# Turning the attention output one tile at a time through the last two heads, and casting its plain blocks on GpSimd

## The chip, the cores and the metric

One core of a Trainium2 chip runs the kernel. The metric is the device time of one execution in microseconds (us). TensorE (PE) multiplies matrices, VectorE (DVE) and ScalarE (ACT) work on SBUF and PSUM, GpSimd (POOL) on SBUF only, and SyncE (SP) issues most of the DMAs. Each engine works through its own instructions in order and waits on semaphores for the others.

## The reference, cut to what matters

```
# attention: 2 batches x 8 heads, 768 tokens, 64 wide; keys of the query's own hash bucket only
scores = np.where(q_bucket == k_bucket, scale * q @ k.T, -1e9)
attn = exp(scores - max) / (sum + 1e-9);  attn_out = attn @ v
x = attn_out.transpose(0, 2, 1, 3).reshape(1536, 512)
# dense mixture: every expert on every token, P from 8 Sinkhorn rounds over x @ w_gate
out = sum_e P[:, e:e+1] * (np.maximum(x @ w1[e], 0) @ w2[e])
# then a routed mixture: one expert a token, on out
```

## The kernel before

**Attention.** The 16 heads are worked in 8 pairs (`pair(j, first, last)`), each of 12 steps `s`, a step being one tile of 128 queries; `i` counts the 96 steps. In step `i` TensorE computes the scores of step `i+2`, transposes the probabilities of step `i` and multiplies those of step `i-1` by V. ScalarE takes the exponential of step `i` (`exp`, L801) and then copies the transposed probabilities of step `i-1` as fp16 (L808). VectorE subtracts for their low halves (`take_probsT_lo`, L1107) and takes the row maximum of step `i+2` (L1113), which the exponential of that step needs. The scores of step `i+2` wait for the exponential of step `i`, since they share a bank of PSUM.

**Turning x.** The dense mixture multiplies with x transposed, in two batches `b` of six tiles of 128 tokens each. `turn_x(t)` has four PE transposes of one tile (L1661) into a PSUM bank, and `take_xf(t)` copies them to `xf` (L843 on ScalarE, L1164 on VectorE). Batch 0 holds heads 0 to 7, which are complete long before the last pair. All of its tiles go through one bank, so each turn waits for the copy of the tile before. In the last pair the steps 6, 7 and 8 turn two tiles each: one between the scores and the transposes, one at the end of the step.

**Seven blocks.** The dense first layer uses Strassen-like sums: seven products per group (`group_product`), of seven sums of W1 blocks and of x blocks. Blocks 0, 4 and 6 of x are plain quarters of `xf`; blocks 2, 1, 3 and 5 are sums that GpSimd makes (`sum_x`, L697 to L705, in that order). Each block needs a high half in fp16 (`x7_hi`, an ACT copy, L854) and a low half (`x7_lo`, a subtraction, L710 on GpSimd for the plain blocks and L1190 on VectorE for the sums). In expert 0 the products of group 0 wait for the blocks of batch 0 one by one, those of group 4 for batch 1.

**Groups.** An expert has 8 groups `g` of 7 products, each product of 6 matmuls (L1722, L1724, L1725). For each group VectorE adds parts out of PSUM: L1275 first (product 5 of the group waits for it), then L1372 for the group before, L1279, L1283, L1286, L1287 and L1290. Batch 1 (tiles 6 to 11) is turned in the groups 0 and 1 of expert 0 through two banks, so tile `t` waits for the copy of tile `t-2`. Its ScalarE work stands in `second_x(g, place)`, between the copies of those groups.

**Splitting W1.** During the attention GpSimd also splits V (`split_v`) and the first expert's W1 (`split_first_w1`), multiplying by a scale that lies in SBUF and is broadcast along the row (`v_scale`, `w_scale`), as a `tensor_tensor`.

## Time and profile before

| | |
|---|---|
| median of 3 runs | 1354.65 us (1350.77 to 1355.5) |
| the profiled execution's own time | 1356.91 us |
| its span, first to last instruction | 1355.1 us |
| PE busy | 97% of the span |
| DVE, ACT, POOL busy | 63%, 42%, 23% |
| granted TensorE clock, mean | 0.993 of full speed |

Busy shares are of the span. With PE at 97%, the time is PE's work and the few stretches in which it waits. The change touches the stretch from about 219 us (last pair of heads) to about 287 us (group 3 of expert 0).

### The profile page before, as it was taken

The page shows a single profiled execution, that of the slowest core. Times are in us where ns is not written, and L with a number is a line of the kernel's source. Part 1 is how long each engine was busy: PE and PEld are TensorE (multiplying, and loading weights), DVE is VectorE, ACT ScalarE, POOL GpSimd, SP SyncE. Part 2 cuts the span into 40 slices and gives each one's busy share as a digit, 9 for nine tenths or more (in the row PEclk, how much of TensorE's full clock was granted, in tenths as well). Part 3 has the DMA queues.
Part 4 walks back from the last instruction along what each step waited for, and adds up shares of the span by engine and source line. Part 5 has one row for each costly group of instructions (what it writes and reads, how often), then busy time and mean ns, then how long its engine had stood idle before and what let it go on. Part 6 is the DMA issues. An engine that isn't in the chain of part 4 may idle for free.

```text
span 1355.1 us, 24730 instructions
## 1 busy us (share of the span) xinstructions
PE 1318.6 (97%) x9435; PEld 763.7 (56%) x9435; DVE 848.4 (63%) x1491; ACT 569.7 (42%) x870; POOL 305.5 (23%) x229
## 2 busy tenths in 40 slices
PE   6999999899999999999999999999999999998987
PEld 3776767665455456445545644654564465556665
DVE  5999999786576247436634742753464275567983
ACT  5999999652134114304312420440242043226662
POOL 4787776522002100300300030030003000121211
PEclk9999999999999999999999999999999999998989
DMA  9345441051011011001101100200110112468940
GB/s 235 95 100 124 111 110 36 37 204 62 1 62 63 1 62 62 0 0 66 58 0 62 62 0 28 72 23 0 62 62 0 62 63 78 180 205 281 342 151 21
DMA packets 51631, 109.84 MB, mean 81 GB/s; under 512 B 5216, under 2 KB 8840, under 8 KB 51568
## 3 DMA queue, kind: packets, MB, share of 16 engines
q1 hardware_dynamic: 48880, 105.40, 24.6%
q0 software_dynamic: 2240, 3.35, 0.7%
q8 instruction: 45, 0.74, 0.2%
q10 hardware_dynamic: 448, 0.19, 0.1%
q14 instruction: 18, 0.15, 0.0%
HBM read 93.57 MB, written 17.34 MB: 82 GB/s over the span
## 4 chain that ended last, share of the span: by engine, by line
PE 89%; DVE 4%; ACT 3%; issue 2%; DMA 1%; SPq 1%; POOL 0%; ACTq 0%; POOLq 0%; DVEq 0%
PE ps L1696 14%; PE ps L1699 14%; PE ps L1700 14%; PE ps L1722 11%; PE ps L1724 11%; PE ps L1725 11%; PE ps L1617 5%; PE ps L1605 2%; PE ps L1607 2%; PE ps L1589 2%; PE ps L1627 1%; PE ps L1629 1%; PE ps L1631 1%; ACT probsT_hi L808 1%; ACT probs L801 1%
## 5 line engine op out<-in xcount | busy, mean ns | idle before, releaser
L1722 PE MATMUL ps<-x_hi,w_hi 128*128 128x384 f16 x896 | 292.3, 326 | 2.3 <-DVE parts L1275 1.2
L1724 PE MATMUL ps<-x_lo,w_hi 128*128 128x384 f16 x896 | 292.3, 326 | 0.0
L1725 PE MATMUL ps<-x_hi,w_lo 128*128 128x384 f16 x896 | 292.3, 326 | 0.0
L1699 PE MATMUL ps<-w_lo,h 128*128 128x512 f16 x768 | 291.2, 379 | 0.0
L1700 PE MATMUL ps<-w_hi,h 128*128 128x512 f16 x768 | 291.2, 379 | 0.0
L1696 PE MATMUL ps<-w_hi,h 128*128 128x512 f16 x768 | 291.1, 379 | 0.0
L1332 DVE SCALAR_TENSOR_TENSOR x<-ps,gate_now,x 128x512 f32<-128x512 f32 x84 | 63.1, 751 | 251.6 <-PE ps L1700 250.6
L938 ACT ACTIVATE x1s<-ps 128x384 f32<-128x384 f32 x64 | 30.4, 475 | 326.5 <-PE ps L1725 326.5
L636 POOL TENSOR_TENSOR wf<-wf 128x1024 f32<-128x1024 f32 x8 | 18.8, 2355 | 633.1 <-PE ps L1725 622.4
L955 ACT ACTIVATE h<-parts 128x1152 f16<-128x1152 f32 x64 | 74.4, 1163 | 140.2 <-DVE parts L1290 140.2
L1700 PEld LDWEIGHTS ps<-w_hi,h 128*128 128x128 f16 x768 | 75.1, 98 | 90.6
L1696 PEld LDWEIGHTS ps<-w_hi,h 128*128 128x128 f16 x768 | 75.7, 99 | 86.3
L1699 PEld LDWEIGHTS ps<-w_lo,h 128*128 128x128 f16 x768 | 75.1, 98 | 86.3
L1722 PEld LDWEIGHTS ps<-x_hi,w_hi 128*128 128x128 f16 x896 | 87.7, 98 | 61.1 <-DVE x_lo L1190 1.7
L1725 PEld LDWEIGHTS ps<-x_hi,w_lo 128*128 128x128 f16 x896 | 87.7, 98 | 57.9
L1724 PEld LDWEIGHTS ps<-x_lo,w_hi 128*128 128x128 f16 x896 | 87.7, 98 | 57.8
L1107 DVE TENSOR_TENSOR probsT_lo<-ps,probsT_hi 128x384 f16<-128x384 f32 x192 | 97.9, 551 | 11.6 <-ACT probsT_hi L808 10.2
L801 ACT ACTIVATE probs<-ps,row_bias,row_scale 128x768 f32<-128x768 f32 x96 | 95.2, 992 | 1.6 <-DVE row_bias L1122 0.8
L1113 DVE TENSOR_REDUCE row_max<-ps 128x1 f32<-128x768 f32 x96 | 91.1, 949 | 3.8 <-PE ps L1607 3.8
L1372 DVE SCALAR_TENSOR_TENSOR h<-parts,h 128x1152 f16<-128x1152 f32 x64 | 86.8, 1356 | 10.4 <-ACT h L955 10.4
L1617 PE MATMUL ps<-const,probs 128*128 128x128 f32 x576 | 87.1, 285 | 3.5 <-DVE probsT_lo L1107 2.3
L808 ACT ACTIVATE probsT_hi<-ps 128x384 f16<-128x384 f32 x192 | 83.4, 490 | 8.6 <-PE ps L1617 7.5
(229 smaller groups left out, 2270.3 us busy)
## 6 DMA issues: line engine op xcount, KB each, us to landing
wf<-w1a SPq DMA_DIRECT2D x32, 512.0 KB, 6.0
w_stage_in<-w2a SPq DMA_DIRECT2D x8, 2048.0 KB, 8.7
w_in<-w1b SPq DMA_DIRECT2D x4, 2048.0 KB, 9.5
w_in<-w2b SPq DMA_DIRECT2D x4, 2048.0 KB, 9.8
w_in_b<-w1b SPq DMA_DIRECT2D x4, 2048.0 KB, 10.0
w_in_b<-w2b SPq DMA_DIRECT2D x4, 2048.0 KB, 10.2
rows<-blank SPq DMA_DIRECT2D x1, 6682.0 KB, 21.5
qk_in<-kT SPq DMA_DIRECT2D x32, 192.0 KB, 4.3
```

Source lines behind the costliest of these rows:

```text
L801: act.activation(probs[r][:, :], psS[r], ACT.Exp, bias=row_bias[:, slot:slot + 1], scale=row_scale[:, slot:slot + 1]).then_inc(probs_ready, 1)
L808: act.activation(probsT_hi[r][:, half * HALF:(half + 1) * HALF], psT[half], ACT.Copy).then_inc(probsT_hi_ready, 1)
L1107: dve.tensor_tensor(probsT_lo[r][:, keys], psT[half], probsT_hi[r][:, keys], ALU.subtract).then_inc(probsT_lo_ready, 1)
L1113: dve.tensor_reduce(row_max[:, slot:slot + 1], psS[r], AX.X, ALU.max).then_inc(max_ready, 1)
L1372: dve.scalar_tensor_tensor(out=h[:, b, 1, i, 1:4, :], in0=now[:, :, :], scalar=0.0, in1=h[:, b, 0, i, 1:4, :], op0=ALU.max, op1=ALU.subtra ...
L1617: last = pe.transpose(psT[half][:, k * P:(k + 1) * P], probs[r][:, keys], ident)
L1696: first = pe.matmul(acc, a_hi, b_hi, start=(m == 0), stop=False)
L1699: pe.matmul(acc, a_hi, b_lo, start=False, stop=False)
L1700: last = pe.matmul(acc, a_lo, b_hi, start=False, stop=(m == n - 1))
L1722: pe.matmul(group_bank(g, role), w_hi, x_hi, start=(opens and kt == 0), stop=False, skip_group_check=not opens)
L1724: pe.matmul(group_bank(g, role), w_hi, x_lo, start=False, stop=False, skip_group_check=not opens)
L1725: last = pe.matmul(group_bank(g, role), w_lo, x_hi, start=False, stop=(kt == 1), skip_group_check=not opens)
```

## The change

It has five parts.

1. Batch 0's tiles are turned one a step, in the steps 0, 2, 3, 4, 5 and 6 of the last pair, each between that step's scores and its transposes. ScalarE takes all of them; VectorE takes none.
2. ScalarE casts only the four sums, at the steps 8 to 11. GpSimd casts the plain blocks 0, 4 and 6 itself and then subtracts.
3. VectorE makes the low halves of the blocks 2 and 1 in the steps 10 and 11, of 3 and 5 after the last step. GpSimd's `normalise` of head 14 moves between the sums.
4. Tiles 10 and 11 of batch 1 are turned after the second product of group 1 (before: after the fifth), and ScalarE takes them one place sooner. In batch 1 GpSimd casts and subtracts block 0, makes the four sums, then casts and subtracts the blocks 4 and 6.
5. The scalings of V and W1 on GpSimd use constants in the instruction (`tensor_scalar`) and no broadcast operand.

```diff
-X_HI = (0, 4, 6, 2, 1, 3, 5)
-X_LO_DVE, X_LO_POOL = (1, 2, 3, 5), (0, 4, 6)
-TAKEN_BY_DVE = (1, 3, 4, 5)
+X_SUMS, X_BLOCKS = (2, 1, 3, 5), (0, 4, 6)
+TURNED_AT = (0, 2, 3, 4, 5, 6)
...
-                pool.tensor_tensor(w7_hi[:, k, :, :], wf[:, k, :, :], scale, ALU.mult).then_inc(w1_hi_ready, 1)
+                pool.tensor_scalar(w7_hi[:, k, :, :], wf[:, k, :, :], W_SCALE, 1.0, ALU.mult, ALU.mult
+                                   ).then_inc(w1_hi_ready, 1)
...
-            def x7_lo_part(b, k):
-                pool.wait_ge(x7_hi_ready, x_hi_count(b, k))
+            def split_x_block(b, k):
+
+                n = len(X_BLOCKS) * b + X_BLOCKS.index(k) + 1
+                pool.wait_ge(xf_ready, QT * b + (QT if k == 6 else QT // 2))
+                pool.tensor_scalar(x7_hi[:, b, k, :, :], x_block(k, b), 1.0, 1.0, ALU.mult, ALU.mult
+                                   ).then_inc(x7_hi_pool, 1)
+                pool.wait_ge(x7_hi_pool, n)
                 pool.tensor_tensor(x7_lo[:, b, k, :, :], x_block(k, b), x7_hi[:, b, k, :, :], ALU.subtract
                                    ).then_inc(x7_lo_pool, 1)
...
             def sum_and_split_x(b):
 
-                x7_lo_part(b, 0)
-                x7_lo_part(b, 4)
+                split_x_block(b, 0)
+                if b == 0:
+                    split_x_block(b, 4)
                 sum_x(b)
-                x7_lo_part(b, 6)
+                if b > 0:
+                    split_x_block(b, 4)
+                split_x_block(b, 6)
...
-                    if last and s >= QT:
-                        first_x(s - QT)
+                    if last and s in TURNED_AT:
+                        take_xf(TURNED_AT.index(s))
+                    if last and s >= 2 * QT - 4:
+                        x7_hi_part(0, s - 2 * QT + 4)
...
-                    if turns_x:
-                        turn_x(2 * (s - QT))
+                    if last and s in TURNED_AT:
+                        turn_x(TURNED_AT.index(s))
...
-                    if turns_x:
-                        turn_x(2 * (s - QT) + 1)
...
+                    if first and g == 1:
+                        turn_x(QT + 4)
+                        turn_x(QT + 5)
                     bank_free(2)
```

On ScalarE, the rows of the last pair of heads around step 6, before: L801 is an exponential, L808 the two copies of transposed probabilities, L843 a turned tile's copy, L854 a cast.

```order
L801 ACTIVATE probs<-ps,row_bias,row_scale 128x768
L808 ACTIVATE probsT_hi<-ps 128x384 x2
L801 ACTIVATE probs<-ps,row_bias,row_scale 128x768
L808 ACTIVATE probsT_hi<-ps 128x384 x2
L843 ACTIVATE xf<-ps 128x4x128
L801 ACTIVATE probs<-ps,row_bias,row_scale 128x768
L808 ACTIVATE probsT_hi<-ps 128x384 x2
L823 ACTIVATE denom<-ps,eps_bias 128x6
L825 ACTIVATE o_sum<-ps 128x384
L843 ACTIVATE xf<-ps 128x4x128
L854 ACTIVATE x_hi<-xf 128x768
```

And the same stretch of the changed kernel (L796 is its exponential, L803 the copies of probabilities, L838 the copy of a turned tile, L844 a cast of a sum):

```order
L796 ACTIVATE probs<-ps,row_bias,row_scale 128x768
L803 ACTIVATE probsT_hi<-ps 128x384 x2
L838 ACTIVATE xf<-ps 128x4x128
L796 ACTIVATE probs<-ps,row_bias,row_scale 128x768
L803 ACTIVATE probsT_hi<-ps 128x384 x2
L838 ACTIVATE xf<-ps 128x4x128
L796 ACTIVATE probs<-ps,row_bias,row_scale 128x768
L803 ACTIVATE probsT_hi<-ps 128x384 x2
L818 ACTIVATE denom<-ps,eps_bias 128x6
L820 ACTIVATE o_sum<-ps 128x384
L796 ACTIVATE probs<-ps,row_bias,row_scale 128x768
```

The copies of tiles now stand one to a step, from the first step of the pair on, each ahead of the next step's exponential; the casts of the plain blocks are gone from this engine.

On VectorE, the end of the last pair and the start of group 0, before: L1190 are the low halves of the sums.

```order
L1107 TENSOR_TENSOR probsT_lo<-ps,probsT_hi 128x384 x2
L1113 TENSOR_REDUCE row_max<-ps 128x1
L1118 TENSOR_SCALAR row_scale<-row_max 128x1
L1122 TENSOR_SCALAR row_bias<-row_max,row_scale 128x1
L1107 TENSOR_TENSOR probsT_lo<-ps,probsT_hi 128x384 x6
L1190 TENSOR_TENSOR x_lo<-x_sums,x_hi 128x768 x4
L1135 TENSOR_SCALAR denom<-ps 128x6
L1129 RECIPROCAL denom<-denom 128x6
L1138 TENSOR_TENSOR x_attn<-ps,denom 128x6x64
L1275 TENSOR_TENSOR parts<-ps,x1s 128x384
```

In the changed kernel (L1086 are the low halves of the probabilities, L1143 those of the sums):

```order
L1086 TENSOR_TENSOR probsT_lo<-ps,probsT_hi 128x384 x2
L1092 TENSOR_REDUCE row_max<-ps 128x1
L1097 TENSOR_SCALAR row_scale<-row_max 128x1
L1101 TENSOR_SCALAR row_bias<-row_max,row_scale 128x1
L1086 TENSOR_TENSOR probsT_lo<-ps,probsT_hi 128x384 x2
L1143 TENSOR_TENSOR x_lo<-x_sums,x_hi 128x768
L1086 TENSOR_TENSOR probsT_lo<-ps,probsT_hi 128x384 x2
L1143 TENSOR_TENSOR x_lo<-x_sums,x_hi 128x768
L1086 TENSOR_TENSOR probsT_lo<-ps,probsT_hi 128x384 x2
L1143 TENSOR_TENSOR x_lo<-x_sums,x_hi 128x768 x2
L1114 TENSOR_SCALAR denom<-ps 128x6
L1108 RECIPROCAL denom<-denom 128x6
```

Two of the four now stand ahead of probabilities that TensorE multiplies.

On GpSimd, batch 1, before: L710 subtracts for a plain block, L697 to L705 are the sums, and the first row holds three subtractions, of block 6 of batch 0 and of the blocks 0 and 4 of batch 1.

```order
L710 TENSOR_TENSOR x_lo<-xf,x_hi 128x768 x3
L697 TENSOR_TENSOR x_sums<-xf 128x768
L700 TENSOR_TENSOR x_sums<-xf,x_sums 128x768
L703 TENSOR_TENSOR x_sums<-xf,x_sums 128x768
L705 TENSOR_TENSOR x_sums<-xf 128x768
L710 TENSOR_TENSOR x_lo<-xf,x_hi 128x768
L724 ISA
```

In the changed kernel (L699 casts, L702 subtracts, L682 to L692 are the sums; the first two rows are block 0 of batch 1, and the views write `x_hi` and `x_lo` for `x7_hi` and `x7_lo`):

```order
L699 TENSOR_SCALAR x_hi<-xf 128x768
L702 TENSOR_TENSOR x_lo<-xf,x_hi 128x768
L682 TENSOR_TENSOR x_sums<-xf 128x768
L685 TENSOR_TENSOR x_sums<-xf,x_sums 128x768
L690 TENSOR_TENSOR x_sums<-xf,x_sums 128x768
L692 TENSOR_TENSOR x_sums<-xf 128x768
L699 TENSOR_SCALAR x_hi<-xf 128x768
L702 TENSOR_TENSOR x_lo<-xf,x_hi 128x768
L699 TENSOR_SCALAR x_hi<-xf 128x768
L702 TENSOR_TENSOR x_lo<-xf,x_hi 128x768
L719 ISA
```

A cast has come in ahead of each subtraction, and behind the sums there are two blocks, four instructions, where there was one instruction.

## Rows read from the trace of the kernel before

**Rows 1.** The page: each engine's busy time, share of the span, instructions.
```profile
PE 1318.6 (97%) x9435; PEld 763.7 (56%) x9435; DVE 848.4 (63%) x1491; ACT 569.7 (42%) x870; POOL 305.5 (23%) x229
```

**Rows 2.** Stretches: length; busy PE, PEld, DVE, ACT, POOL (instructions); clock; DMA share, GB/s.
```profile
233.00:247.50 14.50, 12.31 (x160) 9.79 (x157) 13.16 (x31) 11.75 (x23) 6.60 (x5) 1.00 0.43 146
247.50:257.00 9.50, 7.03 (x87) 5.03 (x88) 7.63 (x9) 6.26 (x12) 7.14 (x4) 1.00 0.01 2
```

**Rows 3.** PE in order of time: start, duration; scores, first turned tile, first product.
```profile
220.49 0.39 PE L1605 MATMUL ps<-K,Q 76*128 76x512 f16 x1
222.86 0.38 PE L1605 MATMUL ps<-K,Q 76*128 76x512 f16 x1
225.09 0.38 PE L1605 MATMUL ps<-K,Q 76*128 76x512 f16 x1
234.01 0.38 PE L1605 MATMUL ps<-K,Q 76*128 76x512 f16 x1
234.67 0.60 PE L1661 MATMUL ps<-const,x_attn 128*128 128x128 f32 x4
236.84 0.39 PE L1605 MATMUL ps<-K,Q 76*128 76x512 f16 x1
243.67 0.38 PE L1605 MATMUL ps<-K,Q 76*128 76x512 f16 x1
252.33 0.33 PE L1722 MATMUL ps<-x_hi,w_hi 128*128 128x384 f16 x1
255.59 0.34 PE L1722 MATMUL ps<-x_hi,w_hi 128*128 128x384 f16 x1 [1.15 <-DVE x_lo L1190]
```

**Rows 4.** ACT in order of time, step 6 of the last pair, and a later cast.
```profile
235.31 0.60 ACT L843 ACTIVATE xf<-ps 128x512 f32<-128x512 f32 x1 [1.12 <-PE ps L1661]
235.80 0.99 ACT L801 ACTIVATE probs<-ps,row_bias,row_scale 128x768 f32<-128x768 f32 x1
246.71 0.84 ACT L854 ACTIVATE x_hi<-xf 128x768 f16<-128x768 f32 x1
```

**Rows 5.** POOL and DVE in order of time, at the end of the attention.
```profile
250.55 1.86 POOL L705 TENSOR_TENSOR x_sums<-xf 128x768 f32<-128x768 f32 x1
252.37 2.35 POOL L710 TENSOR_TENSOR x_lo<-xf,x_hi 128x768 f16<-128x768 f32 x1
251.80 3.73 DVE L1190 TENSOR_TENSOR x_lo<-x_sums,x_hi 128x768 f16<-128x768 f32 x2
```

**Rows 6.** In order of time, group 1 of expert 0: third product, copies of tiles 8, 9.
```profile
264.18 0.33 PE L1722 MATMUL ps<-x_hi,w_hi 128*128 128x384 f16 x1
264.22 1.07 ACT L843 ACTIVATE xf<-ps 128x512 f32<-128x512 f32 x2
```

**Rows 7.** POOL and DVE in order of time, groups 2 and 3 of expert 0.
```profile
269.86 2.17 POOL L697 TENSOR_TENSOR x_sums<-xf 128x768 f32<-128x768 f32 x1
276.83 2.19 POOL L705 TENSOR_TENSOR x_sums<-xf 128x768 f32<-128x768 f32 x1
278.97 1.65 POOL L710 TENSOR_TENSOR x_lo<-xf,x_hi 128x768 f16<-128x768 f32 x1
278.14 0.96 DVE L1294 CAST earlier<-const 128x128 bf16<-128x128 f32 x1
279.02 1.63 DVE L1296 CAST x<-const 128x12 uint32<-128x12 f32 x1
280.63 1.81 DVE L1190 TENSOR_TENSOR x_lo<-x_sums,x_hi 128x768 f16<-128x768 f32 x2
```

**Rows 8.** POOL by line: count, busy us and mean ns, idle before.
```profile
L581 POOL TENSOR_SCALAR marks<-hashed,mark_top,mark_floor 44x768 f16<-44x768 f32 x15 | 14.7, 981 | 11.1 <-ACT hashed L816 10.1 <-issue 1.0
L663 POOL TENSOR_TENSOR w_hi<-wf,w_scale 128x1024 f16<-128x1024 f32 x7 | 13.2, 1893 | 0.3
L604 POOL TENSOR_TENSOR V_hi<-V_in,v_scale 128x384 f16<-128x384 f32 x16 | 13.9, 869 | 34.0 <-PE ps L1631 23.0 <-DMA V_in<-v 10.2 <-POOL marks L581 0.7
```

**Rows 9.** Who PE waited for, 225 to 290 us: total, times, longest.
```profile
PE ps L1722 <- DVE parts L1275: 1.2, 1, 1.2
```

More of the change, by code:

```diff
@@ L348, in x_tile @@
             return xf[:, t // QT, :, (t % QT) * P:(t % QT + 1) * P]
-        def act_tiles(t):
-            return sum(u not in TAKEN_BY_DVE for u in range(t + 1))
-        def dve_tiles(t):
-            return sum(u in TAKEN_BY_DVE for u in range(t + 1))
-        def x_hi_count(b, k):
-            return NP * b + X_HI.index(k) + 1
         def group_bank(g, role):
@@ L683, in _ @@
                 split_first_w1(j - 1)
-            normalise(G - 2)
             pool.wait_ge(v_split, 3 * G)
@@ L1170, in pair @@
                     g, r, q = 2 * j + s // QT, s // QT, s % QT
-                    if last and s in (QT + 1, QT + 2, QT + 3):
-                        take_xf((1, 3, 5)[s - QT - 1])
                     if not (first and s == 0):
@@ L1175, in pair @@
                         take_probsT_lo(i - 1, 1, (s - 1) % 2)
-                    if last and s == QT + 2:
-                        take_xf(4)
+                    if last and s >= 2 * QT - 2:
+                        x7_lo_part(0, X_SUMS[s - 2 * QT + 2])
                     ends_head = q == 1 and not (first and s == 1)
@@ L1667, in pair @@
                     g, r, q = 2 * j + s // QT, s // QT, s % QT
-                    turns_x = last and QT <= s < QT + 3
                     if not (last and s >= 2 * QT - 2):
@@ L1761, in expert @@
                     group_product(g, 0, 1, 4, False)
-                    if first and g < 2:
-                        turn_x(QT + 4 * g)
-                        turn_x(QT + 4 * g + 1)
+                    if first and g == 0:
+                        turn_x(QT)
+                        turn_x(QT + 1)
                     pe.wait_ge(u2_ready, groups_done + 1)
```

80 lines of the change are left out of this document (31 added, 49 removed).

## The prediction

> **What bounds the kernel now.** The page comes first: PE is busy for 97% of the span [rows 1], so only two things can move the time, PE's own work and PE's waits. The change takes nothing from PE: it still turns 12 tiles, and multiplies the same blocks. So I look for waits, in the stretch that the change touches, with the busy time by stretches. PE lacks 2.19 us in 233 to 247.5 and 2.47 us in 247.5 to 257 [rows 2]; from 225 to 290 the list of waits has one of 1.2 us more, for L1275 [rows 9]. Together 5.9 us, 0.43% of the time, is all that the change could win there. The order of PE in time then shows where each loss lies [rows 3].
>
> From 225.09 to 234.01, four steps without a turned tile, a step takes 2.23 us. Step 6, the first with tiles, takes 2.83 (234.01 to 236.84), and the next two take 6.83 together (to 243.67). The first product of expert 0 starts at 252.33. Two products later PE stands, for 1.15 us by the row, until 255.59: it waits for the low half of a sum.
>
> **The turned tiles of batch 0.** What does one tile a step cost? Step 6 of before has its first tile just where the change puts each of its tiles, and the rows follow one another without a gap: scores 0.66 us (234.01 to 234.67), the tile's transposes 0.60, ScalarE's copy at 235.31, the exponential at 235.80 for 0.99, and the next step's scores at 236.84 [rows 3, 4]. ScalarE works in order: it has the copy ahead of the next exponential, and so the exponential can't start before PE has done scores and tile. The chain is 2.83 us against 2.23, so 0.60 a tile, although ScalarE and PE both have time left in a step. Step 0 took 2.37 (220.49 to 222.86), it grows by 0.46. Steps 2 to 5 grow by 4 x 0.60 = 2.4. Step 6 stays. PE is at step 7 about 2.9 us late.
>
> Steps 7 and 8 hold no tile now. Before they took 6.83. Step 1, which like step 7 copies a head's sums, took 2.23 (222.86 to 225.09) [rows 3]; I take 2.3 for step 7, and for step 8, whose ScalarE row has a cast of 0.84 [rows 4] beside the exponential and two copies, 2.4. That gives 2.1 back. From step 9 to the first product it took 8.66 us (243.67 to 252.33). ScalarE now has a cast in each of the steps 9, 10 and 11 where it had two, and VectorE has two low halves of about 0.9 us (1.81 for two [rows 7]) ahead of probabilities that PE waits for. I put 0.3 on it; nothing to 1.5 is open. First product: 2.9 - 2.1 + 0.3 = 1.1 us later.
>
> The wait of 1.15 us after it goes: blocks 2 and 1 have their low halves before the last probabilities are done, block 3 follows 0.9 us later, and PE needs it only after three products. First term: 1.1 - 1.15 = **0.0 us**, with -2.9 and +1.2 as its ends (the tiles free, or the tail 1.5).
>
> **Tiles 10 and 11.** Tile 10 now stands behind two products of group 1, which end at 264.18, and each tile waits for the copy of two tiles before. ScalarE copies tiles 8 and 9 from 264.22 for 1.07 us [rows 6], so the first is there at about 264.8 and the second at 265.3. Unhindered, tile 11 would start by 264.18 + 0.60 = 264.8 at the latest. Nothing of this waits before. Second term: **+0.6 us** (0.5 to 0.8), and ScalarE can't be quicker, since its copies stand behind work of group 0 that keeps its distance to PE.
>
> **GpSimd and VectorE in batch 1.** GpSimd and VectorE hold one another up. At 251.80 VectorE starts two low halves, which take 3.73 us for the 1.81 of the pair at 280.63 [rows 5, 7]. The first can only end after GpSimd's sum (250.55 + 1.86 = 252.41), the second after its subtraction (to 254.72), which itself takes 2.35 for 1.65. In groups 2 and 3 the casts at 278.14 and 279.02 end with GpSimd's instructions too (279.02 and 280.62), and behind them stand the low halves and L1275, for which PE waited 1.2 us [rows 7, 9].
>
> The Trainium skill says the same (GPSIMD Engine Reference, section 8, Key points): GpSimd contends with VectorE instructions that have two SBUF inputs or run in a two-port mode. It speaks against this change, which gives GpSimd three more instructions in each batch; the rows agree with it.
>
> Before, GpSimd is done at 280.62, just as VectorE comes to its two low halves. How long is it busy now? The cast is not in the trace. A tensor_scalar of 768 elements took 0.98 us on 44 partitions [rows 8], a tensor_tensor of the same size up to 1.65; I take 1.0, being the same kind of instruction. By the Trainium skill (the same page, 3.1) one-input work runs at 1.03 cycles an element at 1.2 GHz: an estimate of 0.7 us, which would take 0.9 us from GpSimd's queue. Block 0 can start with tile 8's copy at about 265.3, cast and subtraction end near 268.2, the four sums took 9.1 (269.86 to 278.97) [rows 7] and end near 277.3, and two blocks of 1.0 + 1.65 bring it to 282.6 or, with what VectorE takes, 284. So both low halves of 0.9 fall under a busy GpSimd: each waits for the rest of an instruction, 0 to 1.65, on average about 0.7, so +1.4. The casts of before waited for longer instructions (2.19 and 1.65); now some are of 1.0, -0.4. PE already stands there, so all of it counts. Third term: **+1.0 us** (-0.5 to +2.8).
>
> **What costs nothing.** The scalings with a constant go from 1.89 us and 0.87 [rows 8] to perhaps 1.3 and 0.6. GpSimd is ahead in the attention: it waits for PE 23.0 us in all before L604. If that cover is gone they cost (below). Batch 0's blocks: turned by step 3, the blocks 0 and 4 are cast and subtracted by about 237, the sums start with the sixth copy near 239 and are made by 247, each ahead of ScalarE's cast. Even a cast of 1.65 would leave that so.
>
> **Sum.** 0.0 + 0.6 + 1.0 = +1.6 us. Against the profiled execution's 1356.91 (its span 1355.1) that is 1358.5; it lies 2.3 above the median of the three runs, so on the median 1354.65 + 1.6 = 1356.2 us.
>
> **Rivals.**
> - *The tiles are free.* A step has slack on ScalarE and PE, and if the copy slips into it the 2.9 us do not arise: -1.3 in all, 1353.3 us. For it: one tile is less than the slack of two engines together. Against it: the 2.83 of step 6, which has the same order. 0.20.
> - *Contention rules.* All low halves in batch 1, and those of the steps 10 and 11 too, wait a whole GpSimd instruction: third term 2.8, tail 1.5, +4.6 in all, 1359.2 us. For it: the 3.73. By the rule of the Trainium skill above (GPSIMD Engine Reference, Key points) this is the case to expect. 0.17.
> - *All waits go*, the 5.9 us: 1348.8 us. Against it: the chain and tile 10. 0.04.
> - *GpSimd becomes the bound (slower).* The two-constant multiplication may be dearer than the multiplication with a broadcast operand. A pair of heads has two such instructions on W1 and four on V, 2 x 1.89 + 4 x 0.87 = 7.3 us, and GpSimd waits for PE 23.0 / 8 = 2.9 a pair. From 1.4 times the duration it decides; at 1.6 times it is 4.4 - 2.9 = 1.5 us a pair, 10 us in the seven, 1366 us. Against it: 0.98 for 768. 0.07.
> - *As forecast*, 0 to +3: 0.52.
>
> **How the numbers follow.** The bounds of the terms give -1 to +5 in the likeliest case; the free tiles reach down to 1353, and three runs of the same kernel lie 4.7 us apart. I take 1350.5 to 1361.0, which leaves out the fourth rival, the third, and the ends of the spread. A measurement of this kernel tells about 0.5% (6.8 us) from no change. Faster by that is below 1347.9, which even the third rival doesn't reach: 0.03. Slower by that takes the GpSimd rival or the contention at its worst with the spread: 0.09. Within: 0.88.
>
> **What would show it.** Scores 2.83 us apart in the steps 0 and 2 to 6 (2.23: the tiles are free). First product near 1 us later against the last pair's start, and no wait for a low half behind it. A wait of PE before tile 11 of 0.5 to 0.8. GpSimd busy to about 284 in batch 1, and the wait for L1275 in group 3 of 2 us, not 1.2. A cast on GpSimd of about 1.0 us. I am wrong if casts or constant scalings take over 1.65, or if PE waits at group 4 for a block that GpSimd makes last.

## The result, and the profile after

| | before | changed |
|---|---|---|
| median, 18 runs each | 1354.61 us (1350.77 to 1357.26) | 1358.11 us (1354.67 to 1360.76) |
| ratio, 95% interval | | 1.0025 (1.0016 to 1.0034) |
| profiled execution, its span | 1356.91, 1355.1 us | 1360.46, 1358.6 us |

The change costs 3.5 us, 0.25% of the time. That is within the 0.5% that the prediction called no change, but the interval of the ratio excludes 1, so it is a small loss. The prediction said +1.6.

The page of the changed kernel, each engine's busy time, share and instructions. PE has the 97% of [rows 1] still; GpSimd (POOL) is busy for 16 us less.

```profile
PE 1319.1 (97%) x9435; PEld 764.0 (56%) x9435; DVE 848.0 (62%) x1487; ACT 566.6 (42%) x868; POOL 289.3 (21%) x235
```

PE of the changed kernel in order of time (start, duration). L1577 is the scores (L1605 before), L1634 a turned tile (L1661), L1692 the first product of a block (L1722), L1666 the second layer. These rows answer to [rows 3, 6].

```profile
220.65 0.39 PE L1577 MATMUL ps<-K,Q 76*128 76x512 f16 x1
221.32 0.60 PE L1634 MATMUL ps<-const,x_attn 128*128 128x128 f32 x4
223.49 0.39 PE L1577 MATMUL ps<-K,Q 76*128 76x512 f16 x1 [0.31 <-ACT probs L796]
225.86 0.38 PE L1577 MATMUL ps<-K,Q 76*128 76x512 f16 x1
226.53 0.60 PE L1634 MATMUL ps<-const,x_attn 128*128 128x128 f32 x4
228.70 0.39 PE L1577 MATMUL ps<-K,Q 76*128 76x512 f16 x1 [0.37 <-ACT probs L796]
...
240.13 0.39 PE L1577 MATMUL ps<-K,Q 76*128 76x512 f16 x1 [0.31 <-ACT probs L796]
244.74 0.38 PE L1577 MATMUL ps<-K,Q 76*128 76x512 f16 x1
251.42 1.51 PE L1589 MATMUL ps<-const,probs 128*128 128x128 f32 x6 [1.81 <-DVE probsT_lo L1086]
255.09 0.51 PE L1692 MATMUL ps<-x_hi,w_hi 128*128 128x384 f16 x1
267.47 0.82 PE L1634 MATMUL ps<-const,x_attn 128*128 128x128 f32 x5 [0.52 <-ACT xf L838]
320.07 0.38 PE L1666 MATMUL ps<-w_hi,h 128*128 128x512 f16 x1
```

Three stretches follow from such rows, and the experiments below are read by the same three: the last pair of heads from its first scores to those of step 9 (**steps**), from there to the first product of expert 0 (**tail**), and from it to the first product of the second layer (**first layer**; it starts at 315.23 before). Their sum is the time that the change can touch. The changed kernel was traced a second time, later, with the median of its own in the last table.

| us | steps | tail | first layer | sum |
|---|---|---|---|---|
| before | 23.18 | 8.66 | 62.90 | 94.74 |
| changed | 24.09 | 10.35 | 64.98 | 99.42 |
| changed, second trace | 24.08 | 8.55 | 65.35 | 97.98 |

The sum grows by 4.7 us in one trace and by 3.2 in the other; the medians differ by 3.5.

Who PE waited for in the changed kernel, 220 to 325 us (total, times, longest). Before there was one wait of 1.2 us in the first layer that the list gives [rows 9], beside the low half's 1.15 [rows 3]. The low half is gone. In its place stand a wait of 1.8 us in the tail, two of 0.6 for x1s, one of 1.1 for the bank that L1247 frees (L1275 before) and one of 0.5 for the copies of the tiles 8 and 9.

```profile
PE ps L1589 <- DVE probsT_lo L1086: 3.4, 5, 1.8
PE ps L1577 <- ACT probs L796: 2.0, 6, 0.4
PE ps L1692 <- ACT x1s L917: 1.2, 2, 0.6
PE ps L1692 <- DVE parts L1247: 1.1, 1, 1.1
PE ps L1634 <- ACT xf L838: 0.5, 1, 0.5
```

Stretches of the changed kernel: length, busy time of PE, PEld, DVE, ACT and POOL, the granted clock, then DMA. The first two answer to [rows 2], where the clock was 1.00 in both. Here it is 0.67 in the second, and the short stretches show where: it is full at 250.50 and half, 1.2 in place of 2.4 GHz, from 250.75 on, inside the wait of 1.81 us (249.61 to 251.42), and it is full again by 257.50. The transposes that start there take 1.51 us; the same six took 0.92 at full clock.

```profile
233.00:247.50 14.50, 12.74 (x171) 9.77 (x169) 12.44 (x30) 13.30 (x25) 11.24 (x9) 1.00 0.39 138
247.50:257.00 9.50, 6.87 (x73) 5.47 (x74) 8.78 (x13) 4.37 (x8) 2.40 (x2) 0.67 0.01 2
...
250.25:250.50 0.25, 0.00 (x0) 0.00 (x0) 0.25 (x1) 0.25 (x1) 0.00 (x0) 1.00 0.00 0
250.75:251.00 0.25, 0.00 (x0) 0.00 (x0) 0.25 (x2) 0.13 (x1) 0.00 (x0) 0.50 0.00 0
...
250.00:252.00 2.00, 0.58 (x3) 0.61 (x4) 2.00 (x4) 0.88 (x2) 0.00 (x0) 0.66 0.00 0
252.00:254.00 2.00, 1.92 (x23) 1.70 (x21) 1.67 (x4) 0.98 (x2) 0.00 (x0) 0.50 0.00 0
254.00:256.00 2.00, 1.89 (x21) 1.42 (x22) 1.97 (x5) 0.00 (x0) 0.00 (x0) 0.50 0.03 8
256.00:258.00 2.00, 2.00 (x9) 1.05 (x8) 0.64 (x2) 0.49 (x1) 0.00 (x0) 0.63 0.00 0
```

POOL by line in the changed kernel (count, busy us and mean ns): V's scaling took 869 ns before and W1's 1893 [rows 8], now 540 and 1046; the cast is L699. GpSimd's new instructions are shorter than the ones they replace, and the new cast takes 1.07 in the mean.

```profile
L590 POOL TENSOR_SCALAR V_hi<-V_in 128x384 f16<-128x384 f32 x16 | 8.6, 540 | 38.8 <-PE ps L1603 27.9 <-DMA V_in<-v 10.5 <-POOL A L581 0.2
L648 POOL TENSOR_SCALAR w_hi<-wf 128x1024 f16<-128x1024 f32 x7 | 7.3, 1046 | 0.4
L699 POOL TENSOR_SCALAR x_hi<-xf 128x768 f16<-128x768 f32 x6 | 6.4, 1068 | 17.5 <-ACT xf L838 17.5
```

### The profile page after: what moved, and what is told of

Same layout as the page of the kernel before. It is cut to its first block, busy times and chain, and to the rows that moved or that the text cites. A ratio compares the mean times of both kernels' runs of the same rounds, so it can differ in the third digit from the quotient of the medians.

```text
span 1358.6 us, 24724 instructions
## 1 busy us (share of the span) xinstructions
PE 1319.1 (97%) x9435; PEld 764.0 (56%) x9435; DVE 848.0 (62%) x1487; ACT 566.6 (42%) x868; POOL 289.3 (21%) x235
## 4 chain that ended last, share of the span: by engine, by line
PE 87%; DVE 5%; ACT 3%; issue 3%; DMA 1%; SPq 1%; POOL 0%; ACTq 0%; POOLq 0%; DVEq 0%
PE ps L1666 14%; PE ps L1669 14%; PE ps L1670 14%; PE ps L1692 10%; PE ps L1694 10%; PE ps L1695 10%; PE ps L1589 4%; PE ps L1577 2%; PE ps L1579 2%; PE ps L1561 1%; ACT probsT_hi L803 1%; DVE probsT_lo L1086 1%; ACT probs L796 1%; PE ps L1599 1%; PE ps L1601 1%
## 5 line engine op out<-in xcount | busy, mean ns | idle before, releaser
L1692 PE MATMUL ps<-x_hi,w_hi 128*128 128x384 f16 x896 | 292.7, 327 | 2.3 <-ACT x1s L917 1.2
L1666 PE MATMUL ps<-w_hi,h 128*128 128x512 f16 x768 | 291.0, 379 | 0.0
L1666 PEld LDWEIGHTS ps<-w_hi,h 128*128 128x128 f16 x768 | 75.7, 99 | 86.3
L1692 PEld LDWEIGHTS ps<-x_hi,w_hi 128*128 128x128 f16 x896 | 87.8, 98 | 61.5 <-ACT x1s L917 1.9
L1086 DVE TENSOR_TENSOR probsT_lo<-ps,probsT_hi 128x384 f16<-128x384 f32 x192 | 98.0, 551 | 13.2 <-ACT probsT_hi L803 11.8
L796 ACT ACTIVATE probs<-ps,row_bias,row_scale 128x768 f32<-128x768 f32 x96 | 95.6, 996 | 0.8
L803 ACT ACTIVATE probsT_hi<-ps 128x384 f16<-128x384 f32 x192 | 83.9, 495 | 8.0 <-PE ps L1589 7.1
```

The costliest lines, as they stand in the source:

```text
L796: act.activation(probs[r][:, :], psS[r], ACT.Exp, bias=row_bias[:, slot:slot + 1], scale=row_scale[:, slot:slot + 1]).then_inc(probs_ready, 1)
L803: act.activation(probsT_hi[r][:, half * HALF:(half + 1) * HALF], psT[half], ACT.Copy).then_inc(probsT_hi_ready, 1)
L1086: dve.tensor_tensor(probsT_lo[r][:, keys], psT[half], probsT_hi[r][:, keys], ALU.subtract).then_inc(probsT_lo_ready, 1)
L1666: first = pe.matmul(acc, a_hi, b_hi, start=(m == 0), stop=False)
L1692: pe.matmul(group_bank(g, role), w_hi, x_hi, start=(opens and kt == 0), stop=False, skip_group_check=not opens)
```

## How VectorE and GpSimd pass one another in the tail

VectorE and GpSimd of the changed kernel around step 10, in order of time. VectorE's low half of a sum (L1143) and GpSimd's subtraction (L702) start 0.03 us apart, GpSimd first. GpSimd takes 1.64 us, and VectorE 2.43 for an instruction of 0.95: it ends 0.82 us after GpSimd's. Behind it stand the low halves of the probabilities (250.72), for which PE waits until 251.42.

```profile
248.37 2.43 DVE L1143 TENSOR_TENSOR x_lo<-x_sums,x_hi 128x768 f16<-128x768 f32 x1
250.72 1.01 DVE L1086 TENSOR_TENSOR probsT_lo<-ps,probsT_hi 128x384 f16<-128x384 f32 x2
...
248.34 1.64 POOL L702 TENSOR_TENSOR x_lo<-xf,x_hi 128x768 f16<-128x768 f32 x1
```

The second trace of the same kernel, the same two instructions, and then the first layer's group 2, where they meet again.

```profile
247.74 0.95 DVE L1143 TENSOR_TENSOR x_lo<-x_sums,x_hi 128x768 f16<-128x768 f32 x1
247.78 2.41 POOL L702 TENSOR_TENSOR x_lo<-xf,x_hi 128x768 f16<-128x768 f32 x1
...
280.29 3.25 DVE L1143 TENSOR_TENSOR x_lo<-x_sums,x_hi 128x768 f16<-128x768 f32 x2
283.47 0.54 DVE L1247 TENSOR_TENSOR parts<-ps,x1s 128x384 f32<-128x384 f32 x1
...
280.38 2.35 POOL L702 TENSOR_TENSOR x_lo<-xf,x_hi 128x768 f16<-128x768 f32 x1
```

Now VectorE is first by 0.04 us; it takes its 0.95, GpSimd pays, and nobody waits for GpSimd there. The tail is 8.55 us in this trace and 10.35 in the other: one program, two outcomes, which go with some hundredths of a microsecond in the two starts. Three more kernels below have this order in step 10; in their traces VectorE is first and keeps its 0.95 twice (tiles 10 and 11 late, changed with the pair later) and is second and takes 2.43 once (batch 1 as before). The Trainium skill describes the mechanism (SBUF — State Buffer, Terms): the port pair that the two engines share is held for the whole instruction, and the loser blocks. The traces agree, with the 2.43 for 0.95 and the 2.41 for 1.64: in each the engine that started first kept its own time.

## The experiments

Each kernel is compared with the kernel before on the same chip, the ratio with its 95% interval. All results are in the table at the end of this section.

**Low halves last** (`e1_low_halves_last`). The changed kernel, with the low halves of the blocks 2 and 1 behind the last probabilities instead of in the steps 10 and 11.

```diff
-                    if last and s >= 2 * QT - 2:
-                        x7_lo_part(0, X_SUMS[s - 2 * QT + 2])
...
-            for k in X_SUMS[2:]:
+            for k in X_SUMS:
```

> The changed kernel with one part undone: VectorE makes the low halves of the sums 2 and 1 behind the last probabilities, and not in the steps 10 and 11. Measured on the trace as the time from the first scores of the last pair to the first product of the second layer (before 94.7 us, changed 99.4 us). My theory: a low half that waits for GpSimd's instruction (2.43 us for 0.9) makes PE stand 1.8 us before the last transposes, and the clock falls to half in that gap. Then the way from the last scores to the first product goes from 10.4 to about 8.9 us, the clock stays full, and the stretch is about 97.3 us, 2 us less. Rival: the clock falls in any case, since PE is sparsely used in the last two steps. Then only about 0.5 us comes back, and the granted clock between 250 and 257 us is still well below 1.

The tail is 8.55 us, with no wait above 0.9 in it (the theory had about 8.9). That agrees with the cause but doesn't prove it alone, since the changed kernel has 8.55 too where VectorE wins. The forecast of 97.3 for the sum missed: it is 99.86, because the first layer is longer, 67.24, with a wait of 2.5 us for the bank of L1245 (L1247 with other line numbers), and the clock at half behind it. That wait is the subject of the later runs.

This run also shows why the 1.15 us for a low half went. VectorE makes all four low halves behind the last probabilities here, as the kernel before does, and PE still doesn't wait for one. What is different is GpSimd:

```profile
251.85 3.55 DVE L1143 TENSOR_TENSOR x_lo<-x_sums,x_hi 128x768 f16<-128x768 f32 x4
247.66 1.64 POOL L702 TENSOR_TENSOR x_lo<-xf,x_hi 128x768 f16<-128x768 f32 x1
```

GpSimd is done with batch 0 at 249.30, before the low halves start, and the four take 3.55. Before, GpSimd worked until 254.72, and the first two alone took 3.73 [rows 5].

**Copy behind the exponential** (`e2_copy_behind_exp`). ScalarE copies a turned tile after the next step's exponential, not ahead of it. PE's order is the changed kernel's.

```diff
                     exp(i, s % 4, s % 2)
+                    if last and s - 1 in TURNED_AT:
+                        take_xf(TURNED_AT.index(s - 1))
...
-                    if last and s in TURNED_AT:
-                        take_xf(TURNED_AT.index(s))
```

> The changed kernel with ScalarE's copy of a turned tile moved behind the next step's exponential; nothing else. My theory: a tile costs 0.6 us because the copy, which waits for PE, stands ahead of the exponential for which PE's next scores wait. With the copy behind it steps with a tile go from 2.84 to about 2.25 us, the last scores come 2.9 us sooner, and the stretch falls from 99.4 to about 96.5 us. Rival: the step is bound by PE's own work (scores, tile, transposes, values), which the order on ScalarE does not change: steps stay near 2.8 us and the stretch at 99.4 us.

ScalarE and then PE of this kernel in order of time. The copy (L838) at 223.20 now follows the exponential (L796), whose start no longer waits for the tile.

```profile
222.32 1.00 ACT L796 ACTIVATE probs<-ps,row_bias,row_scale 128x768 f32<-128x768 f32 x1
223.20 0.61 ACT L838 ACTIVATE xf<-ps 128x512 f32<-128x512 f32 x1
...
226.34 0.38 PE L1577 MATMUL ps<-K,Q 76*128 76x512 f16 x1
227.01 0.60 PE L1634 MATMUL ps<-const,x_attn 128*128 128x128 f32 x4
```

A step with a tile takes 2.31 us in place of 2.84, and the steps together 20.38 in place of 24.09: 3.7 us less, and 2.8 less than before the change. The work on PE and ScalarE is the same, so it was the order on ScalarE that cost 0.5 of the 0.6 a tile. The tail is 9.13 (a wait of 1.2 for the last probabilities, behind a low half of 1.47 in step 11). The ratio is 0.9988: below 1, though barely. The sum, 94.85, is 1.7 under the 96.5 expected; 1.2 of that is the tail, 9.13 for the 10.35 of the first trace.

**Tiles 10 and 11 late** (`e3_tile10_late`). The second term alone undone: both tiles are turned where they were before.

```diff
-                    if first and g == 1:
-                        turn_x(QT + 4)
-                        turn_x(QT + 5)
...
-                    if first and g == 0:
-                        turn_x(QT)
-                        turn_x(QT + 1)
+                    if first and g < 2:
+                        turn_x(QT + 4 * g)
+                        turn_x(QT + 4 * g + 1)
```

> The changed kernel with tiles 10 and 11 turned behind the fifth product of group 1 and copied one place later, as before. My theory: the wait of 0.5 us before tile 11 goes and nothing else changes: 98.8 us for the stretch. Rival: the earlier tiles let GpSimd begin its sums of batch 1 sooner, and with them later the GpSimd work runs further into groups 2 and 3 and the waits there grow: 99.4 us or more.

The wait of 0.5 us before tile 11 is gone, and nothing is gained, as the rival had it: the wait for L1247 is 3.2 us here, and the first layer 67.15. The 0.5 was slack to a later wait for the same engines' work. (1.7 of the 67.15 is a second fall of the clock, of which more below.) By its ratio, 1.0043 (1.0026 to 1.0060), this kernel is no better than the changed one.

**Batch 1 as before** (`e4_b1_as_before`). Part 4 of the change undone whole: the tiles late, ScalarE casts the blocks 0, 4 and 6, GpSimd only subtracts, 0 and 4 ahead of its sums.

```diff
+                if b == 0:
                     pool.wait_ge(xf_ready, ...)
                     pool.tensor_scalar(x7_hi[:, b, k, :, :], ...)
...
+                elif (g, place) == (1, 1):
+                    x7_hi_block(0)
+                    x7_hi_block(4)
+                elif (g, place) == (2, 0):
+                    x7_hi_block(6)
```

> The changed kernel with batch 1 wholly as before: tiles 10 and 11 late, ScalarE casts the blocks 0, 4 and 6 of batch 1, GpSimd subtracts 0 and 4 ahead of the sums. My theory: the two waits for ScalarE's copy of product 1 in groups 2 and 3 (0.64 and 0.54 us) come from VectorE standing behind GpSimd instructions (2.23 us for 0.56), and go; so does the 0.5 us before tile 11: 97.3 us for the stretch. Rival: those waits come from the later start of batch 1 against GpSimd, not from its casts: 98.8 us, as without the early tiles alone.

The first layer is 62.75 us: 2.2 to 2.6 less than in the two traces of the changed kernel, with the one wait of 1.1 that the kernel before has. The sum is 97.19, where the theory had 97.3. This trace lost the race in step 10 (tail 10.35, clock at half until 257), so the first 2.5 us of its first layer are at half clock, which costs about 1 (61.75 below, at full clock). The ratio, 1.0016, can't be told from the changed kernel's 1.0025 by the intervals; only the waits in the trace differ clearly.

**Constants only** (`e5_constants_only`). The kernel before with the scalings of part 5 and nothing else.

```diff
-                pool.tensor_tensor(V_hi[r][:, :, 0:D], V_in[r][:, :, :], scale, ALU.mult
+                pool.tensor_scalar(V_hi[r][:, :, 0:D], V_in[r][:, :, :], V_SCALE, 1.0, ALU.mult, ALU.mult
...
```

> The kernel before with the constants in GpSimd's scalings of V and W1, nothing else. My theory: 0 us, since GpSimd waits for PE there; V's scalings take 0.52 for 0.83 us and W1's 1.05 for 1.89. Rival: GpSimd's earlier end moves its collisions with VectorE, or the second batch, and the time moves by over 1 us.

Ratio 1.0010 (0.9997 to 1.0022), the sum 94.98 against 94.74. GpSimd is busy for 282.1 us here, 23 less than before, and that is worth nothing that can be measured: it waited for PE anyway.

**All three** (`e6_all_three`): the edits of the first, second and fourth run together.

> The changed kernel with ScalarE's copy of a tile behind the next exponential, all low halves of the sums behind the last probabilities, and batch 1 wholly as before. If the three costs add (3.7 us for the order of the copies, 1.8 us for the low half that lost against GpSimd, the rest for batch 1), the last pair's first to last scores take 20.4 us, the way from there to the first product 8.6, and from there to the second layer 61.6 with the clock full, since the wait for a low half after the second product is gone: 90.6 us for the stretch against 94.7 before, 4 us less than before, 0.997 of its time. Rival: what is gained early comes back as waits for GpSimd in batch 1, as it did in the last experiments: the last part is 64 us or more and the kernel is no faster than before.

Steps 20.38, tail 8.54, first layer 61.75, in all 90.67, with the clock at full through the three. The median is 1350.89 us, the ratio 0.9973 (0.9959 to 0.9988): faster than both kernels, and the version to keep. 61.75 is also exactly the 62.90 of before less the 1.15 that the low half cost.

**Copy and low halves** (`e7_copy_and_low`): the first two edits, batch 1 as changed. What it has over the run before is the cost of part 4.

> The same without the return of batch 1: GpSimd casts its plain blocks in batch 1, tiles 10 and 11 stand early. My theory: batch 1 on GpSimd is the larger loss. The stretch is 20.4 + 8.6 + 65.3 = 94.3 us, with a wait of about 2.5 us for L1247's sum in group 3 and the clock at half behind it; 3.5 us more than the version with batch 1 as before. Rival: the wait in group 3 hangs on how the last pair ends; then it is under 1.5 us here and the clock stays full.

It is 96.18, with 67.24 in the first layer, where the theory had 94.3 and 65.3: 5.5 us more than with batch 1 as before, and the ratio is 1.0005 against 0.9973, 4.3 us. Stretches of this kernel, columns as above: PE stands in the first, and the clock is at half behind it; and it falls once more at 302 us, with PE busy all the time. That second fall is what the theory lacked. The shortfall from 1, times 2 us each, is 1.7 us in the first group and 1.7 in the second.

```profile
280.00:282.00 2.00, 0.64 (x3) 0.36 (x4) 2.00 (x3) 0.00 (x0) 0.02 (x1) 0.91 1.06 375
282.00:284.00 2.00, 2.00 (x8) 0.93 (x7) 1.74 (x4) 0.00 (x0) 0.00 (x0) 0.50 1.05 377
284.00:286.00 2.00, 2.00 (x11) 1.10 (x10) 1.63 (x4) 0.07 (x1) 0.00 (x0) 0.74 1.05 378
...
302.00:304.00 2.00, 2.00 (x8) 0.98 (x7) 0.24 (x1) 0.49 (x1) 0.00 (x0) 0.53 0.00 0
304.00:306.00 2.00, 2.00 (x9) 1.03 (x8) 0.66 (x2) 0.00 (x0) 0.00 (x0) 0.62 0.00 0
```

**Which half of part 4** (`e8_act_casts_early_tile`, `e9_pool_casts_old_order`). Both have the edits of the first two runs. The one gives the casts of batch 1 back to ScalarE and keeps the tiles 10 and 11 early, so ScalarE casts the blocks 0 and 4 one place later; the other keeps the casts on GpSimd, with block 4 ahead of the sums and the tiles late. The first one's edit on ScalarE, against the run with all three:

```diff
-                elif (g, place) == (1, 2):
+                elif (g, place) == (1, 1):
                     take_xf(QT + 4)
...
-                elif (g, place) == (1, 1):
+                elif (g, place) == (1, 2):
                     x7_hi_block(0)
                     x7_hi_block(4)
```

> Copy behind the exponential and low halves last, as in the run with these two; in batch 1 ScalarE casts the plain blocks 0, 4 and 6 and GpSimd subtracts 0 and 4 where the kernel before has them, but the tiles 10 and 11 are still turned with the second group. Theory (GpSimd's casts behind the sums are what costs): one short wait of about 0.5 us before tile 11, no wait of 2.5 us for a normalised block, no fall of the clock, first expert product to second layer about 62.3 us (61.75 with everything as before, plus 0.5), first scores to second layer about 91.2, ratio to before about 0.998. Rival (the early tile alone makes VectorE and GpSimd collide): a wait of 2 us or more for a block or its low half, 64 us or more for the stretch, ratio about 1.000.

> Copy behind the exponential and low halves last; tiles 10 and 11 late as before; GpSimd casts all plain blocks of batch 1 as in the changed kernel, but block 4's steps stand ahead of the attention sums on GpSimd, where the kernel before has them. Theory (the casts' own work, 0.83 us each on GpSimd and the collisions it brings, makes GpSimd late): the wait of about 2.5 us for the block with an x1s half (or its low half) stays, the clock falls behind it, first expert product to second layer 65 us or more. Rival (it is block 4's place behind the sums that makes it late): no wait above 1.3 us, the stretch about 62 us, first scores to second layer about 91.

The first theory fell: with ScalarE casting and the tiles early, the wait is 3.3 us and the first layer 67.83, as long as with all of part 4. The second held: 2.5 us of wait, 65.11. Either half is enough, so neither the casts' work nor the place of block 4 is the cause by itself. The first of the two doesn't separate the early tiles from the late casts, though: ScalarE's casts of the blocks 0 and 4 come one place later in it, and GpSimd starts on them 16.8 us after the first product, with all three edits 13.2. The rows say what the two have in common. First, with all three edits, the copy of 12 elements that VectorE has ahead of its pair of low halves, the pair, and GpSimd's last subtraction; then the same copy of the changed kernel, where GpSimd was done before it:

```profile
275.20 1.64 DVE L1274 CAST x<-const 128x12 uint32<-128x12 f32 x1
276.81 1.81 DVE L1151 TENSOR_TENSOR x_lo<-x_sums,x_hi 128x768 f16<-128x768 f32 x2
275.16 1.64 POOL L703 TENSOR_TENSOR x_lo<-xf,x_hi 128x768 f16<-128x768 f32 x1
...
285.33 0.17 DVE L1268 CAST x<-const 128x12 uint32<-128x12 f32 x1
```

The pair and the subtraction with ScalarE's casts and early tiles:

```profile
276.95 3.27 DVE L1151 TENSOR_TENSOR x_lo<-x_sums,x_hi 128x768 f16<-128x768 f32 x2
276.91 1.63 POOL L703 TENSOR_TENSOR x_lo<-xf,x_hi 128x768 f16<-128x768 f32 x1
```

And the pair with GpSimd's casts in the old order is 3.25 too. Where GpSimd is done before VectorE comes to the pair, the pair takes 1.81 us; where both are at it at once, 3.25. The first addition with x1s of the next group (L1247 and its like) stands behind the pair on VectorE, and PE waits for it.

GpSimd's last instruction ends, counted from the first product of expert 0 in the same trace (a difference of two rows):

| kernel | GpSimd done | VectorE's pair | longest wait in the first layer | first layer |
|---|---|---|---|---|
| all three | 27.15 | 1.81 | 1.2 | 61.75 |
| batch 1 as before | 28.15 | 1.81 | 1.1 | 62.75 |
| before | 28.29 | 1.81 | 1.2 | 62.90 |
| constants only | 28.52 | 1.81 | 1.4 | 63.13 |
| GpSimd casts, old order | 29.83 | 3.25 | 2.5 | 65.11 |
| copy behind exponential | 30.06 | 3.25 | 2.5 | 65.34 |
| changed, second trace | 30.07 | 3.25 | 2.5 | 65.35 |
| tiles 10, 11 late | 30.19 | 3.25 | 3.2 | 67.15 |
| changed | 30.24 | 1.81 | 1.1 | 64.98 |
| low halves last | 30.28 | 3.25 | 2.5 | 67.24 |
| copy and low halves | 30.28 | 3.25 | 2.5 | 67.24 |
| ScalarE casts, early tiles | 30.62 | 3.27 | 3.3 | 67.83 |

Before, the end of GpSimd's work and the start of the pair lie 0.01 us apart, and so they do with all three edits, where GpSimd is done 1.1 us sooner. That is no measure of slack. VectorE's copy of 12 elements ahead of the pair ends with GpSimd's last instruction, after 1.63 and 1.64 us in place of the 0.17 undisturbed: VectorE was already being held before the change. What part 4 does, in any of its forms, is to end GpSimd's work 1.5 to 2.3 us later than before, and so the pair is held as well.

The first trace of the changed kernel is the exception among the late ones. A second race decides it, in group 2:

```profile
273.15 2.23 DVE L1258 TENSOR_TENSOR parts<-parts 128x384 f32<-128x384 f32 x1
273.13 1.83 POOL L685 TENSOR_TENSOR x_sums<-xf,x_sums 128x768 f32<-128x768 f32 x1
```

GpSimd is first by 0.02 us here, and VectorE takes 2.23 in place of 0.56. In the second trace VectorE is first by 0.01 (269.55 and 269.56) and keeps its 0.56. Having lost 1.67 there and 1.08 in the next group, VectorE comes to the pair only after GpSimd is done; PE's loss is then spread over waits of 0.6, 0.6 and 1.1.

**The pair one place later** (`e10_pair_later`, `e11_after_pair_later`). If the addition is only queued behind the pair, it can go ahead of it.

```diff
                     if g > 0:
                         split_rest(g - 1, groups_done - 1, before)
+                    if first and g == 3:
+                        for k in X_SUMS[:2]:
+                            x7_lo_part(1, k)
...
-                    if first and g in (2, 3):
-                        for k in X_SUMS[2 * (g - 2):2 * (g - 1)]:
+                    if first and g == 3:
+                        for k in X_SUMS[2:]:
```

> The run with the copy behind the exponential and the low halves last, GpSimd's casts and the early tiles 10 and 11 kept, and one edit more: the first two low halves of batch 1's sums are issued by VectorE in group 3, behind the addition of x1s (with whose bank TensorE's product 5 of that group waits) and behind the low half of h, no longer in group 2 ahead of both. Theory (the wait of 2.5 us is that addition queued behind a pair of low halves that took 3.25 us in place of 1.81, since GpSimd's last subtraction starts within 0.1 us of the pair): the wait goes, no fall of the clock around 280, first expert product to second layer 62.3 to 62.9 us against 67.24, ratio to before 0.997 to 0.998. Rival (GpSimd is simply late and TensorE waits elsewhere for the same 2.5 us, in group 3 or 4): the stretch stays above 65 us and the ratio above 0.999.

> The changed kernel with that one edit alone (first pair of low halves of batch 1 behind the addition and the low half of h in group 3). Theory: the stretch from the first expert product to the second layer falls from 65.35 us (changed kernel, second trace) to 62.3 to 62.9; the turned tiles keep their 0.9 us and the race in step 10 its 0 or 1.8 us, so the time is 2.5 to 4 us under the changed kernel's, ratio to before 0.999 to 1.000. Rival (the late GpSimd costs the same elsewhere): ratio 1.002 to 1.003 as the changed kernel.

VectorE and GpSimd with the copy, the low halves and this edit, in order of time: the addition (L1245) goes first, and the pair is 1.82 us.

```profile
279.58 0.56 DVE L1245 TENSOR_TENSOR parts<-ps,x1s 128x384 f32<-128x384 f32 x1
...
281.32 1.82 DVE L1143 TENSOR_TENSOR x_lo<-x_sums,x_hi 128x768 f16<-128x768 f32 x2
...
277.73 1.64 POOL L702 TENSOR_TENSOR x_lo<-xf,x_hi 128x768 f16<-128x768 f32 x1
```

There is no wait of 2.5 us, the clock stays at full, and the ratio of 0.9979 (0.9966 to 0.9991) is where the theory put it, against 1.0005 (0.9991 to 1.0019) without the edit. The first layer missed its bounds by 1.0 us: 63.89, with waits of 0.5, 0.6, 0.6 and, for a low half at group 4, 1.0. The rival has that part of the loss. This trace alone doesn't show that the edit took the wait away: VectorE lost the race of group 2 in it (2.23 us at 267.19, GpSimd first by 0.02), as in the changed kernel's first trace, which had no wait of 2.5 either.

In the changed kernel with the same edit VectorE won that race, and there the wait of 2.5 is gone too, so this trace carries the reading. But it gained less: 64.81 in place of 65.35, waits of 1.2 and 0.6 for low halves at group 4, and a stretch at 0.57 of the clock at 302 us. Its ratio, 1.0010 (1.0000 to 1.0021), is at the upper bound of the theory's 0.999 to 1.000 and overlaps that of the changed kernel. So the edit removes the large wait, but the late engines keep a part of the cost; with batch 1 as before the first layer is still 2.1 us shorter.

| kernel | median (runs) | ratio to before, 95% | steps | tail | first layer | sum |
|---|---|---|---|---|---|---|
| low halves last | 1357.3 (12) | 1.0015 (1.0006 to 1.0024) | 24.07 | 8.55 | 67.24 | 99.86 |
| copy behind exponential | 1353.71 (11) | 0.9988 (0.9978 to 0.9998) | 20.38 | 9.13 | 65.34 | 94.85 |
| tiles 10, 11 late | 1360.61 (6) | 1.0043 (1.0026 to 1.0060) | 24.07 | 8.54 | 67.15 | 99.76 |
| batch 1 as before | 1357.57 (11) | 1.0016 (1.0005 to 1.0028) | 24.09 | 10.35 | 62.75 | 97.19 |
| constants only | 1355.79 (12) | 1.0010 (0.9997 to 1.0022) | 23.18 | 8.67 | 63.13 | 94.98 |
| all three | 1350.89 (12) | 0.9973 (0.9959 to 0.9988) | 20.38 | 8.54 | 61.75 | 90.67 |
| copy and low halves | 1354.98 (12) | 1.0005 (0.9991 to 1.0019) | 20.39 | 8.55 | 67.24 | 96.18 |
| changed, again | 1357.45 (12) | 1.0019 (1.0006 to 1.0031) | 24.08 | 8.55 | 65.35 | 97.98 |
| ScalarE casts, early tiles | 1356.71 (12) | 1.0018 (1.0008 to 1.0027) | 20.38 | 8.55 | 67.83 | 96.76 |
| GpSimd casts, old order | 1356.0 (11) | 1.0007 (0.9996 to 1.0017) | 20.38 | 8.55 | 65.11 | 94.04 |
| pair later | 1352.55 (12) | 0.9979 (0.9966 to 0.9991) | 20.39 | 8.55 | 63.89 | 92.83 |
| changed, pair later | 1356.08 (12) | 1.0010 (1.0000 to 1.0021) | 24.07 | 8.54 | 64.81 | 97.42 |

The changed kernel once more (`after_again`) was meant for its race and its sum:

> The changed kernel once more, for a second profile and for times on the same chip as the others. If the low half of step 10 starts within some 50 ns of GpSimd's subtraction, it may win this time: then it takes 0.95 us, the way from last scores to first product is 8.5 us, and the half clock comes in group 3 and not at the first product. If the order of the two is fixed, it loses again: 2.4 us, 10.4 us, the clock at half from about 251 to 257 us.

The low half won this time: a tail of 8.55, and the half clock in group 3. The ratio, 1.0019, repeats the loss of the first comparison.

## Why the prediction was right, and where it was not

- *The turned tiles.* Right. Forecast were steps of 2.83 us, the first of them +0.46; they are 2.84, 2.84, 2.93, 2.82, 2.84 and 2.84, and the scores of step 7 come 3.1 us later against the start of the pair (2.9 forecast). The steps 7 and 8 gave 2.2 back (2.1). Step 1, without a tile, grew by 0.1 too (2.37 for 2.23). The chain through ScalarE's order is shown by the copy behind the exponential. The rival of free tiles was wrong for this order, and right for another.
- *The tail, +0.3.* Mis-sized, because it is not one number: -0.1 where VectorE wins the race in step 10, +1.7 where it loses. The +1.7 is beyond its end of 1.5, and for another reason than waiting: in the lost case the wait grows by 0.9 us only (0.90 to 1.81), and the clock takes most of the rest (0.59 of it in the six transposes).
- *The low half's wait of 1.15.* It is gone in every kernel with the change to batch 0, but not for the reason given, that the blocks 2 and 1 have their low halves early. With all four behind the last probabilities it is gone as well: what counts is that GpSimd is done with batch 0 before VectorE starts on them.
- *Tiles 10 and 11, +0.6.* The wait for the copy of the tiles 8 and 9 is there (0.52 us). But as a term of the sum it failed: taken away alone, it is paid at the next wait. The two waits, both for engines that are late together, did not add here.
- *GpSimd and VectorE in batch 1, +1.0.* GpSimd was forecast well: busy to about 284, measured 285.33 in a trace that had started 0.16 us later and was 2.8 us behind at the first product, not 1.1. But its end at 280.62 was read as the moment at which VectorE comes to the pair, although VectorE had by then been held for most of the 1.63 us of a small copy. The wait for L1247 was put at 2 us: 2.5 in the second trace, in the first 1.1 with 1.2 more for x1s. But the term of 1.0 was too small. Together with the tiles' 0.6 it stood against 3.2 and 3.6 us (64.98 and 65.35 less 61.75). In the second trace these are the tile's 0.5, 1.3 for the longer wait and about 1.7 for the clock (0.77, 0.50 and 0.87 in the three stretches of 2 us behind it). In the first, the waits make 1.6, as much as forecast, and the fall of the clock that began in the tail costs about 1 (62.75 less 61.75, from the run with batch 1 as before, whose tail is the same); some 0.6 stay unassigned. VectorE's two casts in group 2, which the term had 0.4 shorter, are only 0.1 shorter: they took 1.65 and 0.83 in the second trace, 0.96 and 1.63 before.
- *No clock in the sum.* This is the step that failed. The clock of before was 1.00 throughout the stretch, and its waits were 1.2 us at most. The prediction sized a wait of 2 us for L1275 and never asked what PE runs at behind it. Behind each wait of 2.5 us or more in the first layer the granted clock, summed over the stretches, falls 1.7 us short of full (with ScalarE's casts and early tiles, where PE waited 3.3 us, 3.4 short): that is time beside the wait itself. Around the wait of 1.81 in the tail it is 3.4 short too, of which 0.4 falls on time in which PE stood. Less the clock's 1.7, the +3.2 of the second trace would be +1.5, and less about 3.0 the +4.7 of the first +1.7 (estimates from these rows): the waits were sized about right in total, though not term by term.
- *What costs nothing.* The scalings: right, 1.0010 with an interval that holds 1. The cast on GpSimd takes 0.82 us undisturbed (1.0 forecast, 0.7 by the rate in the Trainium skill, GPSIMD Engine Reference, 3.1) and 1.07 in the mean.
- *The rivals.* The one on contention had the right mechanism and the nearest time, 1359.2 us with a probability of 0.17: the rule of the Trainium skill beside it (GPSIMD Engine Reference, Key points) was borne out where VectorE came second (2.43 in step 10 of the first trace, 3.25 in group 2 of the second), and in neither trace at both places. It too had no clock in it, so its nearness is in part luck.

The whole, on the medians: +3.5 for +1.6. That is inside the range and beyond the 0 to +3 of the case that had 0.52; the range held because it was wide enough for a term that it did not contain. What is not known: how often an execution loses the race in step 10 or the one in group 2, since only profiled executions show it. Of five traces with the changed kernel's order in step 10, two lost.

## What to carry to other kernels

A tile that is "free" for the busiest engine still costs if an engine that works in order puts its copy ahead of the instruction on the chain: put it behind (3.7 us here). Before work is moved onto GpSimd, look at which of its instructions are still to come when VectorE reaches one with two SBUF inputs, and at what waits behind that one. A VectorE instruction that is far longer than its like and ends with GpSimd's is being held already, as the copy of 12 elements was. Here GpSimd ending 2.7 to 3.5 us later than with all three edits cost 3.4 to 6.1 us of the first layer, the falls of the clock included. And give every new wait of PE of about 2 us a second price for the clock behind it.

## What the runs showed of the hardware

- Two instructions of VectorE and GpSimd that start 0.03 to 0.04 us apart end either way: 2.43 and 1.64 us, or 0.95 and 2.41. The same program shows both. VectorE's copies are held too: 1.63 us for 12 elements a partition beside a GpSimd subtraction, 0.17 without one.
- TensorE's clock went to half during or behind waits of 1.81, 2.5, 3.2 and 3.3 us: inside the waits of 1.81 and 3.3, behind the others. It did not behind those of 1.2 us and less in the kernel before, nor behind one of 1.42 in the run with constants only. It fell once more, some 20 us later and with PE busy all the time, in three traces of those with a wait of 2.5 us or more (low halves last, tiles late, copy and low halves), for the same 1.7 us; their first layers are 67.15 to 67.24, where those with one fall and a wait of 2.5 are 65.11 to 65.35. In the changed kernel with the pair later, it fell there alone, some 14 us behind a wait of 1.2. No run here separates the cause of this second fall.
- GpSimd's multiplication by two constants takes 0.54 us for 384 elements a partition, 0.82 for 768 and 1.05 for 1024; with a broadcast operand it took 0.87 for 384 and 1.89 for 1024 [rows 8].
